# Scaling and splitting w_out with ACT and Pool in the prologue of an attention, SoLU and routed-expert kernel

## The reference, cut to what matters

```
attn  = softmax(q_c @ k_c^T / 8) @ v_c          # chunks of 64, 8 batches, 8 heads, 576 positions
x     = attn as rows of 512                     # 4608 tokens
h     = x @ w_in                                # 512 -> 1024
solu  = h * softmax(h)
ln    = (solu - mean) / sqrt(var + 1e-6) * g_ln
x2    = ln @ w_out                              # 1024 -> 512
e     = argmax(x2 @ w_gate)                     # one of 8 experts per token
out   = gate_w * sigmoid(x2 @ w_output_gate)[e] * (relu(x2 @ w1[e]) @ w2[e])
```

## Time and profile before

| | us |
|---|---|
| three runs | 1148.08, 1148.81, 6159.94 |
| median | 1148.81 |
| the profiled execution, its own time | 1147.24 |
| its span, first to last instruction | 1145.5 |
| PE busy | 1080.0 |
| DVE busy | 585.1 |
| ACT busy | 382.1 |
| Pool busy | 216.4 |

### The profile page before, as it was taken

One profiled execution on the slowest core, in us unless ns is written; L12 is line 12 of the kernel. 1 busy time (PEld: TensorE's weight loads), 2 busy tenths in 40 slices (PEclk: granted clock), 3 DMA queues, 4 the chain that ended last, 5 costly groups with the idle time before them and its releaser, 6 DMA issues.

```text
span 1145.5 us, 22549 instructions
## 1 busy us (share of the span) xinstructions
PE 1080.0 (94%) x6180; PEld 896.5 (78%) x6181; DVE 585.1 (51%) x1217; ACT 382.1 (33%) x644; POOL 216.4 (19%) x375
## 2 busy tenths in 40 slices
PE   4899999999999999999992999999999999999695
PEld 3688888888888888888882888888888888888584
DVE  6866767666675767666654333424333332332420
ACT  3433334333333334333330333324333332342321
POOL 2443211202120211202122011111111111111110
PEclk9899999999999999999996999999999999999898
DMA  7541232212221132212001444332423242142000
GB/s 225 183 139 59 62 74 73 63 47 74 73 62 62 60 73 73 64 46 74 29 19 47 120 131 128 126 119 80 124 92 125 77 136 84 54 137 75 28 30 28
DMA packets 57270, 96.70 MB, mean 84 GB/s; under 512 B 15759, under 2 KB 15887, under 8 KB 57233
## 3 DMA queue, kind: packets, MB, share of 16 engines
q1 hardware_dynamic: 47168, 75.60, 21.7%
q0 software_dynamic: 7968, 20.61, 6.1%
q10 hardware_dynamic: 2096, 0.04, 0.1%
HBM read 76.66 MB, written 20.60 MB: 85 GB/s over the span
## 4 chain that ended last, share of the span: by engine, by line
PE 91%; DVE 2%; DMA 2%; issue 1%; ACT 1%; SPq 0%; POOL 0%; ACTq 0%; DVEq 0%; POOLq 0%
PE Y_ps L431 37%; PE H_ps L431 36%; PE T L423 6%; PE S_ps L480 3%; PE X_ps L490 3%; PE L_ps L458 3%; PE X_ps L423 2%; PE S_ps L423 2%; DMA stage<-in_k 1%; ACT x L623 1%; DVE wx L684 1%; DMA stage<-in_moe_w_out 0%; DMA prob<-x_rows,slot_rec 0%; DVE dl L684 0%; POOL route_table L1010 0%
## 5 line engine op out<-in xcount | busy, mean ns | idle before, releaser
L431 PE MATMUL Y_ps<-wx,dh 128*128 (+1 forms) x1216 | 386.3, 399 | 2.7 <-DVE dl L684 2.6
L431 PE MATMUL H_ps<-wx,xh 128*128 (+1 forms) x1216 | 336.5, 399 | 12.2 <-DVE wx L684 8.7
L431 PEld LDWEIGHTS H_ps<-wx,xh 128*128 128x128 f32 x1216 | 225.0, 190 | 57.6 <-issue 11.8
L431 PEld LDWEIGHTS Y_ps<-wx,dh 128*128 128x128 f32 x1216 | 220.1, 188 | 49.5 <-issue 8.1
L431 PE MATMUL Y_ps<-wx,dl 128*128 (+1 forms) x608 | 238.2, 392 | 0.0
L431 PE MATMUL H_ps<-wx,xl 128*128 (+1 forms) x608 | 188.7, 392 | 0.0
L684 DVE TENSOR_TENSOR wx<-stage,wx (+1 forms) x63 | 76.6, 1225 | 156.9 <-ACT wx L637 156.3
L431 PEld LDWEIGHTS H_ps<-wx,xl 128*128 128x128 f32 x608 | 115.0, 189 | 25.1
L431 PEld LDWEIGHTS Y_ps<-wx,dl 128*128 128x128 f32 x608 | 114.1, 188 | 25.4
L564 ACT ACTIVATE stage<-T 64x512 f32<-64x512 f32 x36 | 21.3, 592 | 206.7 <-PE T L423 167.4
L716 DVE TENSOR_REDUCE nmax_h<-H_ps 128x1 f32<-128x1024 f32 x36 | 44.1, 1224 | 86.1 <-PE H_ps L431 86.1
(11 more groups left out here) (161 smaller groups left out, 1252.7 us busy)
## 6 DMA issues: line engine op xcount, KB each, us to landing
stage<-in_moe_w SPq DMA_DIRECT2D x128, 256.0 KB, 3.0
stage<-in_q SPq DMA_DIRECT2D x36, 256.0 KB, 2.9
stage<-in_k SPq DMA_DIRECT2D x72, 128.0 KB, 3.1
stage<-in_v SPq DMA_DIRECT2D x36, 256.0 KB, 3.2
x_rows<-x SPq DMA_DIRECT2D x36, 256.0 KB, 2.0
stage<-in_moe_w_out SPq DMA_DIRECT2D x4, 512.0 KB, 3.9
stage<-in_moe_w_in SPq DMA_DIRECT2D x3, 512.0 KB, 8.5
slot_rec<-route_table SPq DMA_DIRECT2D x40, 2.0 KB, 1.6
```

Of the source, the lines that this page charges most:

```text
L431: i = pe.matmul(acc[:, c0:c0 + HALF], x[:, kk, :], w(part, kk * cols + c0), start=first and x is hi and part == 0, stop=last and x is lo)
```

## The change

Pieces 4 to 7 no longer touch DVE. ACT waits for the load itself and writes `hi` with two activations of 128x512 that carry `g_ln` as a scale from memory (one value per partition). Pool, ahead of its own steps, does for each piece two multiplications of 128x512 in place and a subtraction of 128x1024 (`first_low`), and counts `wout_lo`. The loads of pieces 6 and 7, and the first loads of expert weights, now wait for `wout_lo`. In step 1, PE waits for `wout_lo` before groups 0, 2, 4 and 6 of the second layer, one piece at a time, in place of once for all pieces.

```diff
         HIGH_PIECES = {(-2, "exp"): range(0, 2), (-1, "x"): range(2, 4), (0, "begin"): range(4, 6), (0, "x"): range(6, PIECES)}
-        LOW_PIECES = {(-2, "norm"): range(0, 1), (-1, "pt"): range(1, 2), (-1, "x"): range(2, 4),
-                      (0, "begin"): range(4, 6), (0, "x"): range(6, PIECES)}
+        LOW_PIECES = {(-2, "norm"): range(0, 1), (-1, "pt"): range(1, 2), (-1, "x"): range(2, 4)}
         HOME = (0, 1, 2, 3, 2, 3, 2, 3)
+        USE = (0, 0, 0, 0, 1, 1, 2, 2)
...
@ load_first (SP)
-                    sp.wait_ge(wsplit_lo, i - 1)
+                    if i < KD + 2:
+                        sp.wait_ge(wsplit_lo, i - 1)
+                    else:
+                        sp.wait_ge(wout_lo, i - KD - 1)
...
@ step (SP), s == 0
-                    sp.wait_ge(wsplit_lo, PIECES)
+                    sp.wait_ge(wout_lo, KD)
...
@ step (PE)
-                    if isinstance(s, int) and s == 1:
-                        pe.wait_ge(wsplit_lo, PIECES)
                     for kk in range(3):
+                        if isinstance(s, int) and s == 1 and kk % 2 == 0:
+                            pe.wait_ge(wout_lo, kk // 2 + 1)
                         products(Y_ps, (dh, dl), DM, lambda part, c0: wts(1, part, 1, c0, HALF), kk, kk == 0, False)
...
                     for kk in range(3, KF):
+                        if isinstance(s, int) and s == 1 and kk % 2 == 0:
+                            pe.wait_ge(wout_lo, kk // 2 + 1)
...
@ first_high (ACT)
                 for i in HIGH_PIECES.get((s, place), ()) if isinstance(s, int) else ():
+                    act.wait_ge(wraw_in[HOME[i]], (USE[i] + 1) * 16)
                     if i < KD:
-                        act.wait_ge(wraw_in[i], 16)
+                        act.activation(first_at(0, i), staged[HOME[i]], ACT.Copy).then_inc(wsplit_hi, 1)
                     else:
-                        act.wait_ge(wscaled, i - KD + 1)
-                    act.activation(first_at(0, i), staged[HOME[i]], ACT.Copy).then_inc(wsplit_hi, 1)
+                        act.wait_ge(gl_in, 48)
+                        f = (i - KD) * 2
+                        act.activation(first_at(0, i)[:, 0, :], staged[HOME[i]][:, 0, :], ACT.Copy, scale=gl[:, f:f + 1])
+                        act.activation(first_at(0, i)[:, 1, :], staged[HOME[i]][:, 1, :], ACT.Copy, scale=gl[:, f + 1:f + 2]).then_inc(wsplit_hi, 1)
...
@ first_low (DVE)
-                    for i in range(group.start, group.stop + 1):
-                        if i in group and i >= KD:
-
-                            x, f = staged[HOME[i]], (i - KD) * 2
-                            dve.wait_ge(wraw_in[HOME[i]], 32 + (i - KD) // 2 * 16)
-                            dve.wait_ge(gl_in, 48)
-                            dve.tensor_scalar(x[:, 0, :], x[:, 0, :], gl[:, f:f + 1], None, ALU.mult)
-                            dve.tensor_scalar(x[:, 1, :], x[:, 1, :], gl[:, f + 1:f + 2], None, ALU.mult).then_inc(wscaled, 1)
-                        if i - 1 in group:
-
-                            dve.wait_ge(wsplit_hi, i)
-                            less(first_at(1, i - 1), staged[HOME[i - 1]], first_at(0, i - 1), wsplit_lo)
+                    for i in group:
+                        dve.wait_ge(wsplit_hi, i + 1)
+                        less(first_at(1, i), staged[HOME[i]], first_at(0, i), wsplit_lo)
...
@ Pool
+            def first_low(i):
+
+                f = (i - KD) * 2
+                pool.wait_ge(wsplit_hi, i + 1)
+                for l in range(2):
+                    pool.tensor_scalar(staged[HOME[i]][:, l, :], staged[HOME[i]][:, l, :], gl[:, f + l:f + l + 1], None, ALU.mult).then_inc(wscaled, 1)
+                pool.wait_ge(wscaled, (i - KD + 1) * 2)
+                last = pool.tensor_tensor(first_at(1, i), staged[HOME[i]], first_at(0, i).bitcast(f32), ALU.subtract)
+                last.then_inc(wout_lo, 1)
...
+            for i in range(KD, PIECES):
+                first_low(i)
             steps(pool.Fori, step)
             send(NCH)
```

More of the change, by code:

```diff
@@ L190, in build @@
         wraw_in = [sem(f"wraw_in{i}") for i in range(4)]
-        wscaled, wsplit_hi, wsplit_lo = sems("wscaled wsplit_hi wsplit_lo")
+        wscaled, wsplit_hi, wsplit_lo, wout_lo = sems("wscaled wsplit_hi wsplit_lo wout_lo")
         raw0_in = [sem(f"raw0_in{i}") for i in range(2)]
```

## The result

The changed kernel takes 1152.82 us (median of six runs, 1151.75 to 1154.21) against 1148.24 for the kernel before, run beside it. The ratio of the two is 1.0041, 95% interval 1.0028 to 1.0054: 4.7 us slower, where 1.4 us faster was forecast and 1145.8 to 1151.5 was the range. The time lies above the range, on the side of rival 1, to which I had given 0.20. Of the runs of before, one at 6159.94 is left out of the ratio.

A forecast was written before the change was run, and what follows sets the result against it. PE, busy 94% of the span, bounds the kernel; only its waits in the prologue can shrink. The first layer of tile 2 starts 1.4 us sooner: 1148.81 - 1.4 = 1147.4 us, range 1145.8 to 1151.5.

The forecast's parts named there:

- rival 1: Slower: Pool's multiplication costs 1.19 us, the second layer starts 2.9 us later than before, total 1151.7; chance 0.20.
- the price of Pool's multiplication: Pool's 128x512 multiplication by g_ln, no row to read: taken as 0.57 us, making one piece on Pool 3.65 us.
- the sum: Prologue up to tile 2: its first layer starts 1.4 us sooner, so 1148.81 - 1.4 = 1147.4.
- the lock: Step 0: Pool's subtraction holds the port pair exclusively, so DVE's line 731 ends at 33.0 and 760 acts as started at 41.15.
- theory P: Formed after the result: Pool's multiplication costs 1.55 us, six times on the chain to the second layer; PE's rest costs clock.
- Nothing changes here: Step 1: line 731 waits for Pool again and ends 6.05 us behind the second layer's start, before 6.11.
- Waiting piece by piece: PE's waits ahead of the second layer: all wout_lo counts there at 41.35, so no gain over one wait, no cost.
- PE's clock: First layer of tile 1: shorter rests might end it up to 2 us sooner; counted as nothing.
- The chain itself: Step 0, second half: Pool's piece 5, load 7, ACT's piece 7, squares, exp, softmax; second layer at 43.1 instead of 44.45.
- Rival 2: No change: piece 7 lands after 5.1 us instead of 3.9, gain 0.2, 1148.6 or 1148.9; chance 0.18.
- The port: DVE beside Pool's subtraction: line 731 waits it out, ending 0.56 us behind Pool; lines reading PSUM would not wait.
- The cover of xs_ops: Step 1: Pool's xs_ops of tile 0 move to 41.35 to 43.4; ACT's eviction of Y reads them near 51, 8 us cover.

The follow-up runs named there:

- the forms: Changed kernel with Pool's multiplications swapped per piece for a constant multiplication, a copy, a multiplication to another place and a product; prices only: 1.54 (constant), 0.58 (copy), 1.02 (product).
- the broadcast product: Changed kernel, but Pool multiplies each piece in one 128x1024 elementwise product with g_ln broadcast, replacing two scalar multiplications; 1151.11 us, ratio 1.0013 to the kernel before.

## Why the prediction was wrong

**The failed step is the price of Pool's multiplication**: "I take 0.57", between "0.52" and "1.19". It is 1.55, above the upper bound. I had put the instruction beside the copy, on the ground that both read one tensor; the forms show 0.58 for the copy and 1.55 for the multiplication. Half of a two-input subtraction was no upper bound either, since that form is cheaper. A piece takes 5.5 to 6.0 us, not 3.65; with six multiplications on the chain, as the sum had it, that is 6 x 0.98 = 5.9 us more. With 1.19 rival 1 gave +2.9, and with 1.55 it would give 2.9 + 6 x 0.36 = +5.1 for the start of the second layer; measured were +1.7 (46.16 against 44.45), or +2.2 counted from tile 0. The other 2.9 us are the lock, and here rival 1 and theory P were wrong too: only the four multiplications of pieces 4 and 5 lie ahead of the second layer. The sum held line 760 back behind Pool's subtraction of piece 7, while in fact the softmax ran beside Pool's multiplication of that piece, and the subtraction ended at 47.24 with the second layer under way. The Trainium skill, "GPSIMD Engine Reference", section "Engine selection", has one-input operations at roughly line-rate. The copy on Pool, 0.58 us where DVE's copy of 128x512 takes 0.68, fits that; the multiplication by a scalar, 1.55 us on Pool and 0.48 on DVE, does not, and the measurement decides.

**What the 3.8 us are made of**: the second layer starts 2.2 us later, counted from tile 0; the clock behind the rest costs 2.3 more; and 0.7 comes back in step 1. The last was forecast as "Nothing changes here". In the kernel before, line 731 was held to 2.30 us, and PE then waited for ACT's eviction of Y; in the changed kernel Pool's expert pieces come later (from 50.96), the same line takes 0.75, and that wait is gone. Before, then after:

```profile
53.83 0.66 PE L423 MATMUL T<-ident,x 128*128 128x128 f32 x4 [0.64 <-ACT x L623]
```

```profile
49.96 0.75 DVE L730 TENSOR_SCALAR cen<-cen,nmean 128x1024 f32<-128x1024 f32 x1
```

That rival 1's formula with the true price, +5.1 for the second layer, comes near the 4.7 measured for the whole kernel is luck: it has neither the clock nor this gain in it, and holds a wait that did not come.

**Waiting piece by piece** "gives nothing" was wrong for the same reason. With Pool late, it lets the second layer start 1.2 us sooner than one wait for all pieces does.

**PE's clock**, "I count it as nothing", was the second term missed. I looked only at the rests that would get shorter, and 731 and X_ps did come sooner. The rest ahead of the second layer grew to 6 us, and the clock behind it cost 2.3 us, the larger part of the loss. Rival 1 had priced the late start without what the rest does to PE.

**The chain itself was right**: Pool's piece 5, load 7, ACT's piece 7, squares, exp, softmax, second layer. Giving pieces 6 and 7 a place of their own moved the second layer by 7 us with Pool's work unchanged. ACT's pair was forecast at 1.3 and takes 1.34. Rival 2 did not come: the loads of w_out land 3.3 to 4.4 us after their issue, median 3.4, where the sum had 3.9.

**The port** was right in kind. Line 731 (730 in the changed kernel) met Pool's subtraction at 29.72 and ended 0.55 behind Pool's end (30.18), but waited 0.26 us instead of 1.35, since Pool's late schedule had it meet the tail. That is luck too, and makes 1.1 of the 1.8 us by which the first layer of tile 1 beat its forecast (3.2 us sooner, counted from tile 0, where 1.4 was forecast); for the rest, piece 5 was ready at 25.3 and not 26.5, and PE started X_ps at 27.19 and not 28.35. The 128x8 tensor_scalar, a half sentence in rival 2, was the one that cost: 1.9 us with the broadcast product. Line 760 (759 in the changed kernel) did not wait: 0.69 us at 44.21, beside Pool's multiplication. The rule of the Trainium skill, "SBUF — State Buffer", "Who interferes with whom", agrees with the runs for Pool's subtraction (0.75 became 2.30, 0.17 became 2.10) and not for its multiplication by a scalar, beside which DVE was held for a fraction of it or not at all.

**The cover of xs_ops** was read off one of its readers. The eviction of Y is not the only one: DVE's reciprocal and ACT's squares of the next tile wait for it too. In the changed kernel it is done at 49.13, 1.5 us ahead of the reciprocal at 50.62, not 8; in the kernel with own staging places and Pool's work as in the change that cover is gone.

**In the expert phase** the prediction had the change cost nothing. Some 1.4 us of difference (mean of four profiled executions each) are there, with no cause shown.

## What to carry to other kernels

Before work moves to an engine, find a row of that very form of instruction on that engine; if there is none, the range must be open upwards, because the count of inputs does not set the price. A load that waits for its staging place hands one engine's slowness to every engine that stands in order behind that load, so look at what else that engine's stream holds: a place of its own for two pieces gave back 1.5 us counted to tile 3 (4.0 counted to tile 2, and 2.5 of them lost again), taking the work off Pool 6.0 of 39.2, and both with a better order 8.7. Price a late start together with PE's clock behind the rest, and count up to a place from which the kernels run alike. When a queue of work goes ahead of a short chain, list all readers of that chain.

## What the hardware showed

- Pool, 128x512 in fp32, with DVE out of its way: multiplication by a scalar 1.54 to 1.57 us, product of a tensor with itself 1.02, copy 0.58. A product with g_ln broadcast takes 1.89 for 128x1024, a subtraction of two tensors 2.35 to 2.40.
- A DVE instruction of 0.17 us on 128x8 elements took 2.10 beside Pool's subtraction and ended with it. Beside Pool's multiplication by a scalar DVE waits less: 0.49 for the same instruction at 43.45, while Pool's second multiplication still ran to 44.79, and 0.69 for line 759, its full speed. Beside Pool's copy DVE waits too: line 760 at 54.40 in the kernel before takes 1.22 and ends 0.54 behind the copy.
- PE at the lower clock level behind a rest of 6 us took 4.13 us for what it does in 2.26 otherwise. The same code behind rests of 16 and 8.7 us had its clock back after different times in different kernels, 1.4 us apart in sum, and by up to 0.6 us in executions of one kernel.
